# Causal convolution and two feed-forward layers in one fused kernel: the next tile's convolution moved to other slots, and another warm-up of TensorE

## The chip, the cores and the metric

One Trainium2 chip, one core. The metric is the device time of one launch in microseconds; the times are a median of runs. The other numbers come from one execution that was recorded by the profiler.

## The reference

A softmax-weighted causal filter of 7 taps per head runs over 4 sequences of 4096 positions of width 192 (8 heads of 24 channels). Its output goes through two layers, each with a wide hidden part of 2048; all is float32.

```
w = softmax(weight)                          # [8 heads, 7 taps]
a[b,s,h,:] = sum_k w[h,k] * x_pad[b,s+k,h,:] # 6 zeros ahead of each sequence
h = a.reshape(16384,192) @ w_in1             # 192 -> 2048
y = (h * cos(h)) @ w_out1                    # 2048 -> 192
h = y @ w_in2
out = (h * clip(h + 3, 0, 6) / 6) @ w_out2
```

## The kernel before

**Tiles, phases, slots.** The 16384 positions are cut into 32 tiles of 512. A tile has a phase of layer 1 (L1) and later a phase of layer 2 (L2). A phase has 8 slots (q = 0 to 7); a slot makes 2 of the 16 chunks of 128 hidden units. The order of phases is: tile 0 in L1, then for k = 1 to 31 a "turn" of L1 of tile k followed by L2 of tile k-1, then L2 of tile 31. Turns 2 to 30 are a hardware loop (`Fori`) on every engine. `Phase` tuples say what a phase does besides its own layer (`turn_phases`, line 292): `result` is the tile whose output it turns for the store, `convolved` the tile for which it makes the convolution.

**TensorE (PE).** Every operand is split into a high and a low part (the float32r type), and products of 64 rows, one in the lower and one in the upper half of the array, run side by side. A slot has 19 such pairs, 38 matmuls in all (`lower`, `upper`, lines 412 and 438): it makes the hidden chunks of slot q in `h_ps` and mixes the gated chunks of slot q-3 (`LAG`) into `acc` and `acc_tail`. `h_ps` has two buffers, so slot q starts with a wait for the gate of slot q-2 (line 419 and on, `g_ready`); slot 0 of a phase also waits for both low parts of its source (`source_waits`, `lo_ready`).

**ScalarE (ACT) and VectorE (DVE).** In L1 a slot is a chain of both: ACT copies `h_ps` to `pre` with rounding, DVE subtracts (`fraction`, L628), ACT takes the sine, DVE multiplies (`gated`, L639), ACT makes `g_hi`, GpSimd (POOL) makes `g_lo`. In L2 it is ACT (Relu), DVE (L642), ACT, POOL. Each engine works its queue in program order.

**The convolution of the next tile** is DVE's, between these. `load_x` on SyncE (SP) fetches 512 positions into `x_in` and `x_in_tail` by 6 DMAs; `turn_x(i)` waits for them (`x_loaded`) and transposes both (L657, L658) into `xT`; `put_halo` copies the 6 positions ahead (L672, L673); `conv_taps` has 14 steps, 7 taps for the 128 main and for the 64 tail channels, into `in_f` and `in_ftail` (L683, L687). Then ACT splits the high parts (`split_high`) and DVE the low ones (L695, L700). In the kernel before all of it stands in the L2 phase of a turn: transposes and halo in slot 0, three steps in each of the slots 1 to 4, two in slot 5, the split in slot 6 (`SPLIT_SLOT`), and `turn_result` (L664, L665) in slot 7 (`TURN_SLOT`).

**SP.** One queue of DMA issues, in program order. `load_x(i)` waits until tile i-1 has been transposed (`x_turned`); `store(i)` waits for the transposes of `turn_result(i)` (`o_turned`). In the loop, before:

```
with sp.Fori(2, TILES - 1) as k:
    load_x(k + 1)
    store(k - 2)
```

**Start.** The loads of the weights, the convolution of tile 0 on DVE, and on PE a warm-up of 10 products (`warm_up`, line 494) that starts once 9 of the 14 steps of tile 0 are done.

Of the kernel before, what the change touches and what calls it, by code (L numbers as in the profile page):

```python
# [14 lines left out]
P = 128  # L15
TOK = 512
LAG = 3
WARM_PRODUCTS = 10
WARM_STEP = 9
G_BUFS = 4  # L20
TWO_PI = float(np.float32(2 * np.pi))
HALF_PI = float(np.float32(np.pi / 2))
# [4 lines left out]

Phase = namedtuple("Phase", "layer tile base before number result convolved conv_from rate setup source")  # L30


def conv_moe_kernel(nc, x, weight, w_in1, w_out1, w_in2, w_out2, out):
# [17 lines left out]
    TILES = B * SEQ // TOK  # L51
# [42 lines left out]
    with ctx:  # L94
# [6 lines left out]
        def sem(name):  # L101
            return ctx.enter_context(nc.semaphore(name))
# [85 lines left out]
        w_exp = sem("w_exp")  # L188
        head_step = sem("head_step")
        taps_spread = sem("taps_spread")  # L190
        taps_ready = sem("taps_ready")
        const_ready = sem("const_ready")

# [55 lines left out]

        STEPS = [(t, part) for t in range(TAPS) for part in (0, 1)]  # L250
        DRAIN_SLOT = LAG
        SPLIT_SLOT = SLOTS - 2
        TURN_SLOT = SLOTS - 1
        TURNS = 19
        STEPS_AHEAD = 4
        L1, L2 = 0, 1
        SPLIT_EARLY = {"hi": 1, "twin": 2, "tail": 4, "low_main": 2, "low_tail": 5}
        SPLIT_AFTER_DRAIN = {"hi": 4, "twin": 4, "tail": 5, "low_main": 5, "low_tail": 6}
# [13 lines left out]
        def result_turn(ph):  # L272


            return ph.number if ph.before == L2 and ph.layer == L2 else ph.number - 1
# [5 lines left out]
        def splits_of(ph):  # L281
# [4 lines left out]
                return ph.tile  # L286
            return ph.tile + 1 + (ph.source == L2)

        def first_phase():
            return Phase(L1, 0, 0, None, 0, None, 1, 1, 2, 0, L2)  # L290

        def turn_phases(k):

            base = 2 * SLOTS * k - SLOTS
            first = isinstance(k, int) and k == 1
            last = isinstance(k, int) and k == TILES - 1
            return [Phase(L1, k, base, L1 if first else L2, 2 * k - 1, None, None, None, None,
                          1 if first else None, L1),
                    Phase(L2, k - 1, base + SLOTS, L1, 2 * k, None if first else k - 2,
                          None if last else k + 1, 1, 3, 2 if first else None, L2)]  # L300

        def last_phase():
            return Phase(L2, TILES - 1, END - SLOTS, L2, 2 * TILES - 1, TILES - 2, None, None, None, None, L1)

        def splits_last(ph, q):

# [4 lines left out]
        @block.sync  # L311
        def _(sp):
            def load_x(i):

                if not isinstance(i, int) or i > 0:
                    sp.wait_ge(x_turned, 2 * i)
                for b in range(BLOCKS_D):
                    sp.dma_start(chip_block(x_in, x_in_tail, b), dram_block(x_blocks, i, b)).then_inc(x_loaded, 16)

            def load_block(b):  # L320
                for dst, src in loads_of(b):
                    sp.dma_start(dst, src).then_inc(staged[buffer_of(b)], 16)

            def store(i):

                sp.wait_ge(o_turned, 2 * (i + 1))
                for b in range(BLOCKS_D):
                    sp.dma_start(dram_block(out_blocks, i, b),
                                 chip_block(o_blk, o_blk_tail, b)).then_inc(o_stored, 16)

            sp.dma_start(w_soft[:, :], weight).then_inc(w_loaded, 16)
            load_x(0)
            for b in range(6):
                load_block(b)
            load_x(1)
            for b in (6, 7):
                sp.wait_ge(wlo_done, b - 5)
                load_block(b)
            for b in (8, 9):
                sp.wait_ge(wlo_done, b - 1)  # L340
                load_block(b)
            load_x(2)
            for b in range(10, 2 * BLOCKS):
                sp.wait_ge(wlo_done, b - 1)
                load_block(b)
            with sp.Fori(2, TILES - 1) as k:
                load_x(k + 1)
                store(k - 2)
            for i in range(TILES - 3, TILES):
                store(i)  # L350
            sp.wait_ge(o_stored, 16 * (BLOCKS_D * TILES + 1))

        @block.tensor
        def _(pe):
# [121 lines left out]
            def phase(ph):  # L476
                for q in range(SLOTS):
                    left = mix_of(ph, q - 1) if q > 0 else None
                    if q == 0 and ph.setup != 0:
                        left = ph.before, 1 - pair_of(ph), SLOTS - LAG - 1  # L480
                    for i in range(TURNS):
                        lower(i, ph, q, ph.base + q, mix_of(ph, q))
                        upper(i, ph, q, ph.base + q, mix_of(ph, q), left)

            def last_mixes():
# [5 lines left out]
                for i in range(3):  # L491
                    upper(i, None, None, None, None, (layer, pair, SLOTS - 1))

            def warm_up():

                pe.wait_ge(whi_done, 1)
                pe.wait_ge(conv_step, WARM_STEP)
                for _ in range(WARM_PRODUCTS):
                    pe.matmul(h_ps[:, 1, TOK:W], win_hi[L1][:, 0:P], win_hi[L1][:, 0:TOK], start=True, stop=True)

            UP, LOW = slice(0, DT), slice(DT, P)
            spread_taps()
# [1 line left out]
            phase(first_phase())  # L504
            for ph in turn_phases(1):
                phase(ph)
            with pe.Fori(2, TILES - 1) as k:
                for ph in turn_phases(k):
                    phase(ph)
            for ph in turn_phases(TILES - 1):  # L510
                phase(ph)
            phase(last_phase())
            last_mixes()

# [1 line left out]
        def _(act):  # L516
# [54 lines left out]
            def phase(ph):  # L571
                for q in range(SLOTS):
                    slot = ph.base + q
                    if ph.setup == 0 and q < 2:
                        act.wait_ge(wlo_done, 3 + q)
                    before_gate(ph.layer, q, slot)
                    if ph.layer == L1:
                        cosine(q, SLOTS * ph.tile + q)
                    if ph.convolved is not None and q == SPLIT_SLOT:
                        act.wait_ge(conv_step, len(STEPS) * (ph.convolved + 1))  # L580
                        split_high(L1, L1)
                    if splits_last(ph, q):
                        act.wait_ge(acc_read, ph.number)
                        split_high(L2, L1)
                    high_part(q, slot, ph.setup != 0 or q >= G_BUFS)
                    if q == DRAIN_SLOT and ph.before is not None:
                        copy_low(ph.before, 1 - pair_of(ph), ph.base, ph.number)
                    if ph.layer == L1 and ph.setup != 0:
                        if q == hands_over(ph)["hi"]:
                            act.wait_ge(acc_read, 1 if ph.setup == 1 else ph.number - 1)  # L590
                            split_hi(L2, L2)
                        if q == hands_over(ph)["twin"]:
                            split_twin(L2, L2)
                        if q == hands_over(ph)["tail"]:
                            split_tail(L2, L2)
                    if ph.setup in SPLIT_IN and q in SPLIT_IN[ph.setup]:
                        weight_high(SPLIT_IN[ph.setup][q])
# [12 lines left out]
            phase(first_phase())  # L610
            for ph in turn_phases(1):
                phase(ph)
            with act.Fori(2, TILES - 1) as k:
                for ph in turn_phases(k):
                    phase(ph)
            for ph in turn_phases(TILES - 1):
                phase(ph)
            phase(last_phase())
            copy_low(L2, pair_of(last_phase()), END, 2 * TILES)

# [1 line left out]
        def _(dve):  # L622
# [80 lines left out]
            def phase(ph):  # L703
                for q in range(SLOTS):
# [7 lines left out]
                    else:  # L712
                        gated(L2, q, slot, None, True)
                    if ph.convolved is not None:
                        if ph.setup != 0 and q == 0:
                            turn_x(ph.convolved)
                            put_halo(ph.convolved)
                        n = (q - ph.conv_from) * ph.rate + (STEPS_AHEAD if ph.setup == 0 else 0)
                        if q >= ph.conv_from:
                            for m in range(n, min(n + ph.rate, len(STEPS))):  # L720
                                conv_taps(ph.convolved, m)
                        if q == SPLIT_SLOT:
                            split_low_main(L1, L1, ph.convolved - 1)
                            split_low_tail(L1, L1, ph.convolved - 1)
                    if q == DRAIN_SLOT and ph.before is not None:
# [10 lines left out]
                        split_low_tail(L2, L1, TILES - 1)  # L736
                    if ph.result is not None and q == TURN_SLOT:
                        turn_result(ph.result, result_turn(ph))

            dve.memset(half_pi[:, :], HALF_PI).then_inc(const_ready, 1)  # L740
            dve.memset(three[:, :], 3.0).then_inc(const_ready, 1)
# [27 lines left out]
            split_low_tail(L1, L2, 0)  # L769
            turn_x(1)  # L770
            put_halo(1)
            for n in range(STEPS_AHEAD):
                conv_taps(1, n)
            phase(first_phase())
            for ph in turn_phases(1):
                phase(ph)
            with dve.Fori(2, TILES - 1) as k:
                for ph in turn_phases(k):
                    phase(ph)
            for ph in turn_phases(TILES - 1):  # L780
                phase(ph)
            phase(last_phase())
            dve.wait_ge(o_turned, 2 * (TILES - 1))
            drain_acc(L2, pair_of(last_phase()), END, 2 * TILES)
# [66 lines left out]
```

## Time and profile before

| what | value |
|---|---|
| median of 3 runs | 2374.57 us (2373.44 to 2374.64) |
| the profiled execution | 2375.52 us, its span 2373.8 us |
| PE busy | 2286.3 us (96%), 19470 matmuls |
| DVE busy | 1851.5 us (78%) |
| ACT busy | 1705.8 us (72%) |
| POOL busy | 1468.8 us (62%) |
| DMA | 32.94 MB, mean 14 GB/s |

Busy times are shares of the span. PE overlaps its matmuls, so its busy time doesn't tell how dense they are; for that one counts them in a stretch. The chain of work that ended last gives PE 44% and DVE 19% of the span, and 22% to "issue", where nothing that the profile shows was waited for.

### The profile page before, as it was taken

What the parts mean: (1) busy time and instruction counts of PE and PEld (TensorE: products, weight loads), DVE (VectorE), ACT (ScalarE), POOL (GpSimd) and SP (SyncE); (2) the same over time, 40 slices, a digit from 0 to 9 for tenths busy, and PEclk for the clock granted to TensorE, in tenths of its full rate; (3) what the DMA queues carried; (4) which work ended last, traced back from release to release, by engine and by line L of the source; (5) the groups of instructions that cost most, each with busy time, mean ns of one, the idle gap of its engine ahead of it and who ended that gap; (6) DMA issues with size and microseconds to landing.
All of it is one profiled execution on the core that took longest, in us unless ns stands there. A gap on an engine that the chain in (4) does not pass through costs nothing.

```text
span 2373.8 us, 57021 instructions
## 1 busy us (share of the span) xinstructions
PE 2286.3 (96%) x19470; PEld 1997.7 (84%) x19470; DVE 1851.5 (78%) x2509; ACT 1705.8 (72%) x2836; POOL 1468.8 (62%) x1059
## 2 busy tenths in 40 slices
PE   5899999999999999999999999999999999999998
PEld 4789798888889888888898888998788988888886
DVE  8688877888877888777888778887778887788853
ACT  5876777766777667777667777677776677776674
POOL 6766666566566666566666665665666666656664
PEclk9999999999999999999999999999999999999999
DMA  4100000000000000000000000000000000000001
GB/s 109 37 8 15 0 13 13 13 13 7 7 13 13 13 13 0 13 13 13 13 9 4 13 13 13 13 0 13 13 13 13 12 1 13 13 13 13 2 7 21
DMA packets 208238, 32.94 MB, mean 14 GB/s; under 512 B 203088, under 2 KB 207184, under 8 KB 208208
## 3 DMA queue, kind: packets, MB, share of 16 engines
q1 hardware_dynamic: 208208, 32.53, 7.8%
q8 instruction: 20, 0.33, 0.1%
q14 instruction: 10, 0.08, 0.0%
HBM read 19.92 MB, written 12.58 MB: 14 GB/s over the span
## 4 chain that ended last, share of the span: by engine, by line
PE 44%; issue 22%; DVE 19%; POOL 9%; ACT 4%; DVEq 1%; POOLq 0%; SPq 0%; DMA 0%; ACTq 0%
PE h_ps L374 18%; PE acc L381 16%; PE acc_tail L388 11%; POOL g_lo L794 9%; DVE in_ftail L687 6%; DVE gate L642 5%; DVE in_f L687 4%; DVE in_f L683 1%; DVE in_tail L700 1%; ACT in_tail L558 1%; DVE in_ftail L651 1%; ACT in_hi L552 1%; ACT in_twin L555 1%; ACT pre L525 1%; ACT g_hi L540 0%
## 5 line engine op out<-in xcount | busy, mean ns | idle before, releaser
L794 POOL TENSOR_TENSOR g_lo<-gate,g_hi 128x512 fp32r<-128x512 f32 x1024 | 1428.9, 1417 | 857.1 <-ACT g_hi L540 855.7
L381 PE MATMUL acc<-g_hi,wout 64*128 64x512 f32 x4096 | 1429.9, 389 | 1.7 <-POOL g_lo L794 1.7
L374 PE MATMUL h_ps<-in_hi,win_hi 64*128 64x512 f32 x2048 | 808.3, 395 | 60.8 <-DVE in_tail L700 46.5
L540 ACT ACTIVATE g_hi<-gate 128x512 fp32r<-128x512 f32 x1024 | 613.7, 631 | 326.4 <-DVE gate L642 275.6
L381 PEld LDWEIGHTS acc<-g_hi,wout 64*128 64x128 f32 x4096 | 756.2, 185 | 66.4 <-issue 3.1
L388 PE MATMUL acc_tail<-g_lo,wout 64*128 64x512 f32 x2048 | 807.4, 394 | 0.0
L388 PE MATMUL acc_tail<-g_hi,wout 64*128 64x512 f32 x2048 | 805.6, 393 | 0.0
L374 PE MATMUL h_ps<-in_lo,win_hi 64*128 64x512 f32 x2048 | 803.2, 392 | 0.0
L374 PE MATMUL h_ps<-in_hi,win_lo 64*128 64x512 f32 x2048 | 800.3, 391 | 0.0
L381 PE MATMUL acc<-g_lo,wout 64*128 64x512 f32 x2048 | 800.2, 391 | 0.0
L374 PE MATMUL h_ps<-in_tail,wtail_hi 64*128 64x512 f32 x2048 | 798.1, 390 | 0.0
L628 DVE TENSOR_TENSOR pre<-pre,h_ps 128x512 f32<-128x512 int32 x512 | 334.6, 684 | 289.5 <-ACT pre L523 288.5
L374 PEld LDWEIGHTS h_ps<-in_hi,win_hi 64*128 64x128 f32 x2048 | 379.1, 185 | 109.8 <-issue 44.7
L525 ACT ACTIVATE pre<-h_ps,three 128x512 f32<-128x512 f32 x512 | 337.2, 683 | 163.8 <-PE h_ps L374 163.1
L642 DVE SCALAR_TENSOR_TENSOR gate<-pre,h_ps 128x512 f32<-128x512 f32 x512 | 332.6, 676 | 126.2 <-ACT pre L525 126.1
L388 PEld LDWEIGHTS acc_tail<-g_lo,wout 64*128 64x128 f32 x2048 | 376.5, 184 | 32.9
L374 PEld LDWEIGHTS h_ps<-in_hi,win_lo 64*128 64x128 f32 x2048 | 378.2, 185 | 27.6
L381 PEld LDWEIGHTS acc<-g_lo,wout 64*128 64x128 f32 x2048 | 376.3, 184 | 29.6
L374 PEld LDWEIGHTS h_ps<-in_lo,win_hi 64*128 64x128 f32 x2048 | 379.2, 185 | 24.8
L388 PEld LDWEIGHTS acc_tail<-g_hi,wout 64*128 64x128 f32 x2048 | 379.3, 185 | 24.5
L374 PEld LDWEIGHTS h_ps<-in_tail,wtail_hi 64*128 64x128 f32 x2048 | 378.6, 185 | 22.4
L533 ACT ACTIVATE pre<-pre,half_pi 128x512 f32<-128x512 f32 x512 | 349.1, 717 | 65.4 <-DVE pre L628 56.2
(72 smaller groups left out, 2359.3 us busy)
## 6 DMA issues: line engine op xcount, KB each, us to landing
x_in<-in_x SPq DMA_DIRECT2D x128, 64.0 KB, 2.2
out_dram<-o_blk SPq DMA_DIRECT2D x128, 64.0 KB, 1.8
blk_tail<-in_x SPq DMA_DIRECT2D x64, 64.0 KB, 2.2
out_dram<-blk_tail SPq DMA_DIRECT2D x64, 64.0 KB, 1.8
stage<-in_moe_w_out SPq DMA_DIRECT2D x6, 384.0 KB, 3.3
stage<-in_moe_w_in SPq DMA_DIRECT2D x3, 512.0 KB, 3.5
stage<-in_moe_w_in SPq DMA_DIRECT2D x6, 256.0 KB, 4.3
gate<-in_moe_w_out SPq DMA_DIRECT2D x2, 384.0 KB, 11.0
```

The costliest lines, as they stand in the source:

```text
L374: return pe.matmul(chunk_of(h_ps, q, half), w, x, start=start, stop=stop)
L381: return pe.matmul(acc[pair][:, :], wout[layer][rows, 2 * q + half, cols], g[rows, :], start=start, stop=stop)
L388: return pe.matmul(acc_tail[pair][:, :], wout[layer][rows, 2 * q + half, P:2 * P], g[rows, :], start=start, stop=stop)
L525: i = act.activation(p, h, ACT.Relu, bias=three[:, 0:1])
L533: act.activation(p, p, ACT.Sin, bias=half_pi[:, 0:1], scale=-TWO_PI).then_inc(cos_ready, 1)
L540: act.activation(chunk_of(g_hi, q, half), chunk_of(gate, q, half), ACT.Copy).then_inc(ghi_ready, 1)
L552: act.activation(in_hi[to][:, :], in_f[layer][:, :], ACT.Copy).then_inc(hi_ready[to], 1)
L555: act.activation(in_twin[to][DT:P, :], in_ftail[layer][:, :], ACT.Copy).then_inc(twin_ready[to], 1)
L628: dve.tensor_tensor(p, p.bitcast(I32), chunk_of(h_ps, q, half), ALU.subtract).then_inc(frac_ready, 1)
L642: dve.scalar_tensor_tensor(out=g, in0=p, scalar=6.0, in1=h, op0=ALU.min, op1=ALU.mult).then_inc(g_ready, 1)
L687: ins = dve.scalar_tensor_tensor(out=dst[:, :], in0=src[:, t:t + TOK], scalar=taps[0:rows, part, t:t + 1], in1=dst[:, :], op0=ALU.mult, op ...
L794: pool.tensor_tensor(chunk_of(g_lo, q, half), chunk_of(gate, q, half), chunk_of(g_hi, q, half).bitcast(F32), ALU.subtract).then_inc(glo_re ...
```

## The change

The transposes of a tile go to slot 7 of a phase (a new field `turned` of `Phase`): in the L2 phase of turn k it is tile k+2, right after `turn_result(k - 2)`. Its halo is put in slot 0 of the next L1 phase, its first four steps in the slots 1, 4, 6 and 7 of that phase, the other ten in the slots 0 to 4 of the L2 phase that follows (2, 2, 2, 1 and 3). `SPLIT_SLOT` is 5 instead of 6 (6 in the first phase). On SP the fourth load stands ahead of the loop, and in the loop the store comes first and then the load of tile k+2. The loops run to 29; turn 30 is written out. The warm-up waits for 7 steps instead of 9 and for two weight blocks instead of one, and issues 84 products of 64 rows, in pairs of lower and upper rows, instead of 10 of 128 rows.

```diff
-WARM_STEP = 9
+WARM_STEP = 7
+WARM_SERIES = 8
-Phase = namedtuple("Phase", "layer tile base before number result convolved conv_from rate setup source")
+Phase = namedtuple("Phase", "layer tile base before number result turned convolved setup source")
-        SPLIT_SLOT = SLOTS - 2
+        SPLIT_SLOT = SLOTS - 3
         TURN_SLOT = SLOTS - 1
+        CONV_FIRST = [4, 4, 6, 8, 10, 12, 14, 14, 14]
+        CONV = {0: [0, 0, 1, 1, 1, 2, 2, 3, 4], 1: [4, 6, 8, 10, 11, 14, 14, 14, 14]}
-        STEPS_AHEAD = 4
+        def conv_range(ph, q):
+            done = CONV_FIRST if ph.setup == 0 else CONV[ph.layer]
+            return range(done[q], done[q + 1])
+        def splits_convolved(ph, q):
+            return ph.convolved is not None and (ph.layer == L2 or ph.setup == 0) and q == split_slot(ph)
+        def split_slot(ph):
+            return SPLIT_SLOT + 1 if ph.setup == 0 else SPLIT_SLOT
         def first_phase():
-            return Phase(L1, 0, 0, None, 0, None, 1, 1, 2, 0, L2)
+            return Phase(L1, 0, 0, None, 0, None, 2, 1, 0, L2)
...
-            return [Phase(L1, k, base, L1 if first else L2, 2 * k - 1, None, None, None, None,
-                          1 if first else None, L1),
-                    Phase(L2, k - 1, base + SLOTS, L1, 2 * k, None if first else k - 2,
-                          None if last else k + 1, 1, 3, 2 if first else None, L2)]
+            more = None if last else k + 1
+            late = isinstance(k, int) and k + 2 >= TILES
+            return [Phase(L1, k, base, L1 if first else L2, 2 * k - 1, None, None, more, 1 if first else None, L1),
+                    Phase(L2, k - 1, base + SLOTS, L1, 2 * k, None if first else k - 2, None if late else k + 2,
+                          more, 2 if first else None, L2)]
...
@@ SyncE
-            with sp.Fori(2, TILES - 1) as k:
-                load_x(k + 1)
+            load_x(3)
+            with sp.Fori(2, TILES - 2) as k:
                 store(k - 2)
-            for i in range(TILES - 3, TILES):
+                load_x(k + 2)
+            for i in range(TILES - 4, TILES):
                 store(i)
@@ TensorE
+            def warm_unit(rows, moving):
+                dst = h_ps[:, 1, TOK:W] if rows is UP else acc[1][:, :]
+                return pe.matmul(dst, win_hi[L1][rows, HALF_FF - P:HALF_FF], moving[L1][rows, 0:TOK],
+                                 start=True, stop=True)
             def warm_up():
-                pe.wait_ge(whi_done, 1)
+                pe.wait_ge(whi_done, 2)
                 pe.wait_ge(conv_step, WARM_STEP)
-                for _ in range(WARM_PRODUCTS):
-                    pe.matmul(h_ps[:, 1, TOK:W], win_hi[L1][:, 0:P], win_hi[L1][:, 0:TOK], start=True, stop=True)
+                for _ in range(WARM_PRODUCTS + WARM_SERIES):
+                    for rows in (LOW, UP):
+                        warm_unit(rows, win_hi)
+                for _ in range(WARM_SERIES):
+                    warm_unit(LOW, win_hi)
+                    warm_unit(UP, wtail_hi)
+                for _ in range(WARM_SERIES):
+                    for rows in (LOW, UP):
+                        warm_unit(rows, win_hi).then_inc(warmed, 1)
+                for _ in range(WARM_SERIES):
+                    for rows in (LOW, UP):
+                        pe.wait_ge(whi_done, 2)
+                        warm_unit(rows, win_hi)
@@ ScalarE
-                    if ph.convolved is not None and q == SPLIT_SLOT:
+                    if splits_convolved(ph, q):
@@ VectorE
                     if ph.convolved is not None:
-                        if ph.setup != 0 and q == 0:
-                            turn_x(ph.convolved)
+                        if ph.layer == L1 and ph.setup != 0 and q == 0:
                             put_halo(ph.convolved)
-                        n = (q - ph.conv_from) * ph.rate + (STEPS_AHEAD if ph.setup == 0 else 0)
-                        if q >= ph.conv_from:
-                            for m in range(n, min(n + ph.rate, len(STEPS))):
-                                conv_taps(ph.convolved, m)
-                        if q == SPLIT_SLOT:
+                        for m in conv_range(ph, q):
+                            conv_taps(ph.convolved, m)
+                        if splits_convolved(ph, q):
                             split_low_main(L1, L1, ph.convolved - 1)
                             split_low_tail(L1, L1, ph.convolved - 1)
...
                     if ph.result is not None and q == TURN_SLOT:
                         turn_result(ph.result, result_turn(ph))
+                    if ph.turned is not None and q == TURN_SLOT:
+                        turn_x(ph.turned)
...
-            for n in range(STEPS_AHEAD):
+            for n in range(CONV_FIRST[0]):
                 conv_taps(1, n)
```

## Rows read from the trace of the kernel before

**Rows 1.** Waits of PE: engine line, what for; us in total, times, longest.

```profile
PE h_ps L374 <- DVE in_tail L700: 46.5, 33, 7.1
PE h_ps L374 <- DVE gate L642: 13.6, 30, 0.5
```

**Rows 2.** PE in order of time: start, duration, line, out<-in, [idle before <-releaser].

```profile
1019.21 0.48 PE L374 MATMUL h_ps<-in_hi,win_hi 64*128 64x512 f32 x1 [1.11 <-DVE in_tail L700]
...
1052.13 0.39 PE L374 MATMUL h_ps<-in_hi,win_hi 64*128 64x512 f32 x1
...
1056.52 0.39 PE L374 MATMUL h_ps<-in_hi,win_hi 64*128 64x512 f32 x1
...
1091.59 0.49 PE L374 MATMUL h_ps<-in_hi,win_hi 64*128 64x512 f32 x1 [1.13 <-DVE in_tail L700]
```

**Rows 3.** DVE and POOL in order of time, slots 2 and 3 of an L2 phase.

```profile
1069.31 0.73 DVE L687 SCALAR_TENSOR_TENSOR in_ftail<-xT_tail,taps,in_ftail 64x512 f32<-64x512 f32 x1
1069.98 1.78 DVE L687 SCALAR_TENSOR_TENSOR in_f<-xT,taps,in_f 128x512 f32<-128x512 f32 x1
...
1069.59 3.32 POOL L794 TENSOR_TENSOR g_lo<-gate,g_hi 128x512 fp32r<-128x512 f32 x2 [2.34 <-ACT g_hi L540]
```

**Rows 4.** Waits of SP's queue; then the page's DMA issues (KB each, us to landing).

```profile
SPq L328 <- DVE blk_tail L665: 2025.4, 32, 102.1
...
blk_tail<-in_x SPq DMA_DIRECT2D x64, 64.0 KB, 2.2
```

**Rows 5.** SP's DMA issues in order of time, around a loop end: start, duration.

```profile
1025.31 0.86 SPq L328 DMA_DIRECT2D out_dram<-blk_tail  x2
1026.98 1.94 SPq L318 DMA_DIRECT2D x_in<-in_x  x4
1029.10 0.88 SPq L318 DMA_DIRECT2D blk_tail<-in_x  x2
```

**Rows 6.** DVE in order of time: end of an L2 phase, then L1 slots 2 and 5.

```profile
1021.92 0.71 DVE L665 STREAM_TRANSPOSE blk_tail<-sum_tail 64x512 f32<-64x512 f32 x1
...
1032.58 1.28 DVE L628 TENSOR_TENSOR pre<-pre,h_ps 128x512 f32<-128x512 int32 x2 [1.71 <-ACT pre L523]
1034.07 1.30 DVE L639 TENSOR_TENSOR gate<-pre,h_ps 128x512 f32<-128x512 f32 x2 [0.20 <-ACT pre L533]
...
1046.65 1.28 DVE L628 TENSOR_TENSOR pre<-pre,h_ps 128x512 f32<-128x512 int32 x2 [1.70 <-ACT pre L523]
```

**Rows 7.** PE and DVE where the last phase, which has no convolution, ends.

```profile
2354.97 0.39 PE L388 MATMUL acc_tail<-g_lo,wout 64*128 64x512 f32 x1
...
2357.07 0.71 DVE L665 STREAM_TRANSPOSE blk_tail<-sum_tail 64x512 f32<-64x512 f32 x1
```

**Rows 8.** DVE in order of time: both transposes of a tile of x.

```profile
1060.16 0.70 DVE L657 STREAM_TRANSPOSE xT<-x_in 128x512 f32<-128x512 f32 x1
1060.79 0.66 DVE L658 STREAM_TRANSPOSE xT_tail<-blk_tail 64x512 f32<-64x512 f32 x1
```

**Rows 9.** Stretches: busy (count) of PE, PEld, DVE, ACT, POOL; PE clock; DMA.

```profile
68.77:72.50 3.73, 0.61 (x5) 0.18 (x1) 3.55 (x4) 3.68 (x8) 3.73 (x4) 0.84 0.36 105
72.50:78.10 5.60, 5.56 (x26) 4.45 (x28) 2.58 (x4) 3.90 (x6) 3.42 (x3) 0.50 0.00 0
...
110.20:113.50 3.30, 0.40 (x4) 0.00 (x0) 3.00 (x4) 2.96 (x6) 3.30 (x4) 1.00 0.00 0
```

**Rows 10.** PE, then DVE, in order of time: the start.

```profile
17.99 4.60 PE L499 MATMUL h_ps<-win_hi 128*128 128x512 f32 x10 [13.28 <-DVE in_f L687]
29.66 0.79 PE L374 MATMUL h_ps<-in_hi,win_hi 64*128 64x512 f32 x1 [7.07 <-DVE in_tail L700]
...
13.77 0.73 DVE L687 SCALAR_TENSOR_TENSOR in_f<-xT,taps,in_f 128x512 f32<-128x512 f32 x1
...
34.72 0.73 DVE L687 SCALAR_TENSOR_TENSOR in_ftail<-xT_tail,taps,in_ftail 64x512 f32<-64x512 f32 x1
...
37.09 0.69 DVE L628 TENSOR_TENSOR pre<-pre,h_ps 128x512 f32<-128x512 int32 x1 [1.03 <-ACT pre L523]
```

More of the change, by code:

```diff
@@ L190, in conv_moe_kernel @@
         taps_spread = sem("taps_spread")
+        warmed = sem("warmed")
         taps_ready = sem("taps_ready")
@@ L296, in turn_phases @@
             last = isinstance(k, int) and k == TILES - 1
-            return [Phase(L1, k, base, L1 if first else L2, 2 * k - 1, None, None, None, None,
-                          1 if first else None, L1),
-                    Phase(L2, k - 1, base + SLOTS, L1, 2 * k, None if first else k - 2,
-                          None if last else k + 1, 1, 3, 2 if first else None, L2)]
+            more = None if last else k + 1
[3 more added lines that the diff above has]
+                          more, 2 if first else None, L2)]
         def last_phase():
-            return Phase(L2, TILES - 1, END - SLOTS, L2, 2 * TILES - 1, TILES - 2, None, None, None, None, L1)
+            return Phase(L2, TILES - 1, END - SLOTS, L2, 2 * TILES - 1, TILES - 2, None, None, None, L1)
         def splits_last(ph, q):
@@ L506, in _ @@
                 phase(ph)
-            with pe.Fori(2, TILES - 1) as k:
+            with pe.Fori(2, TILES - 2) as k:
                 for ph in turn_phases(k):
                     phase(ph)
-            for ph in turn_phases(TILES - 1):
-                phase(ph)
+            for k in (TILES - 2, TILES - 1):
+                for ph in turn_phases(k):
+                    phase(ph)
             phase(last_phase())
@@ L612, in _ @@
                 phase(ph)
-            with act.Fori(2, TILES - 1) as k:
+            with act.Fori(2, TILES - 2) as k:
                 for ph in turn_phases(k):
                     phase(ph)
-            for ph in turn_phases(TILES - 1):
-                phase(ph)
+            for k in (TILES - 2, TILES - 1):
+                for ph in turn_phases(k):
+                    phase(ph)
             phase(last_phase())
@@ L776, in _ @@
                 phase(ph)
-            with dve.Fori(2, TILES - 1) as k:
+            with dve.Fori(2, TILES - 2) as k:
                 for ph in turn_phases(k):
                     phase(ph)
-            for ph in turn_phases(TILES - 1):
-                phase(ph)
+            for k in (TILES - 2, TILES - 1):
+                for ph in turn_phases(k):
+                    phase(ph)
             phase(last_phase())
```

## The prediction

> **What bounds the kernel now.** I read four views, in this order: the page, the waits of PE, PE in order of time over one turn, and then the queues of DVE and SP over the same turn. The waits name what PE stands for in the loop: the low part of the next tile's source, 33 times, and the gate of L2, 30 times [rows 1]. PE in order of time gives the price. A slot without a wait takes 1056.52 - 1052.13 = 4.39 us [rows 2], which is 0.116 us for each of its 38 matmuls. A turn of 16 such slots would be 70.3 us, and it is 1091.59 - 1019.21 = 72.4 us [rows 2]. So PE bounds the kernel, all but some 2.1 us of each turn, and those go to DVE: in the L2 phase a slot with three steps of the convolution is longer than PE's 4.39 us, since a step takes 0.73 us alone and 1.78 us where a `g_lo` of POOL runs already [rows 3]. DVE falls behind, the gate of slot 5 is 0.5 us late, and the split in slot 6 ends 1.1 us after PE wants it. 30 turns (k = 1 to 30) have this loss, about 62 us in all. That is the most that the moved steps can win in the loop.
>
> **Steps, halo and split.** Of the 14 steps an L2 slot now holds two at most in slots 0 to 2, one beside the drain, and three in slot 4. Two gates (2 x 0.6 us) and two steps, one alone and one behind POOL, make 1.2 + 0.7 + 1.7 = 3.6 us, under 4.39. Slot 4 has 1.2 + 0.7 + 2 x 1.7 = 5.3 us, so DVE ends it 0.9 us late; the gate may come almost two slots after its chunk before PE needs the buffer, and the split starts then, in slot 5, over one slot ahead of PE's demand. In L1 a slot has four DVE instructions of 0.65 us, 2.6 us of 4.39, and gets one thing more: the halo (four copies), a step, a low split, or the drain. A lone step starts before POOL's `g_lo` of that slot and takes 0.73 us, and POOL has the room to give it back. I price all this at nothing, and take the whole loss of 2.1 us off a turn. If the cover fails, it is by a step that starts behind POOL and costs 1 us more in L1; bounds for a turn: 2.1 us won, down to 1.0 us.
>
> **The transposes.** This is the part that I expect to decide. In the L2 phase of turn k, slot 7, DVE runs `turn_result(k - 2)` and then `turn_x(k + 2)`, which waits for the load of tile k+2. SP's program in turn k is `store(k - 2)` and then `load_x(k + 2)`, and the store waits for exactly that `turn_result`. SP does stand at that wait nearly all the time, 2025 us of the span [rows 4], so nothing lets the load go earlier. Before, the store stood there too, but the load behind it was needed only half a turn later. Now DVE waits, with its queue blocked, for six store issues, six load issues and a landing.
>
> Its length, from a turn of the kernel before, where the same issues follow each other: the result's transposes end at 1021.92 + 0.71 = 1022.63 [rows 6]; the last load issue ends at 1029.10 + 0.88 = 1029.98 and so starts at about 1029.6 [rows 5]; it lands 2.2 us later [rows 4], at 1031.8. That is 9.2 us. Between the store's last issue (ends 1026.17) and the load's first (1026.98) lies the loop's branch [rows 5], which is no longer there; of these 0.8 us I take 0.4 off. The wait is 8.8 us (bounds 8.3 and 9.3).
>
> Now against PE. Let T be the start of L1 slot 0. In the last phase, which has no convolution and therefore no lag, the slot after slot 7 starts at 2354.97 and the result's transposes end at 2357.78 [rows 7], at T + 2.8. The load has landed at T + 11.6, both transposes (1.3 us from 1060.16 to 1061.45 [rows 8]) end at T + 12.9. Only then can DVE take the first fraction of L1 slot 0, and from a first fraction to the end of a first gate it is 1034.07 + 0.69 - 1032.58 = 2.2 us [rows 6]: T + 15.1. PE needs that gate to start slot 2 at T + 8.8. With 0.1 us for the release, PE stands 6.4 us (bounds 5.7 and 7.1). ACT and POOL wait for the same fraction; nothing else on PE's queue can pass.
>
> **The clock.** After a stall of 3.7 us the granted clock fell, and the next 5.6 us of dense work were granted 0.50, the 1.2 GHz level: 26 matmuls instead of 5.6 / 0.116 = 48, so 5.6 - 26 x 0.116 = 2.6 us lost [rows 9]. A stall of 3.3 us left the clock at 1.00 [rows 9]. 6.4 us is longer than both, so I add 2.6 us a turn (bounds 0 and 3.5). It falls on slot 2 and a part of slot 3, where the chain of ACT and DVE has no lead to give.
>
> The Trainium skill, "TensorE: Matmul & The Clock Gate", section "Why this matters for your kernels", says the same of idle gaps between bursts of matmuls, and by it too each turn would pay anew; 110.2 to 113.5 us shows that a gap has to be long enough. The same notes, "DMA: Bandwidth & Descriptors", section "Rules for kernel authors", ask that a DMA be issued early and its semaphore be waited for late, so that the fixed cost overlaps. The trace before does that (DVE never waits for a load in the loop), and the change undoes it; that page's fixed cost of about 2 us for a DMA is close to the 2.2 us measured here from issue to landing, and an estimate with 2.0 would be 28 x 0.2 = 6 us lower.
>
> **How many turns.** The wait exists where a load stands behind a store: k = 2 to 29, 28 turns. In turn 1 tile 3 is loaded ahead of the loop, and in turns 30 and 31 nothing is transposed. Each of the 28 turns changes by + 6.4 + 2.6 - 2.1 = + 6.9 us, which is + 193; turns 1 and 30 win 2.1 each, - 4.
>
> **The start.** The warm-up now starts when step 7 is done, at 14.5 us instead of 18.0 [rows 10]. Its 42 pairs take 0.43 us each at 1.2 GHz and 0.23 us at 2.4 [rows 9, 2]: 9.7 us if all were fast, 18 us if all were slow; with 13 slow ones, as in the 5.6 us above, 12.3 us, to 26.8. PE's first real product waits for the split until 29.66 anyway [rows 10], so the warm-up is hidden unless it is slow throughout (then 2.9 us late). Before, the first phase began at the lower level. At the higher one its first chunk comes 2 us earlier, but DVE is at the steps of tile 1 until 35.45 and takes the first fraction then, as it does now; only the 1.03 us that it waited for the second chunk goes [rows 10]. Behind this the chain of ACT and DVE sets the pace of the first phase. I take - 1 us (bounds - 4 and + 3). The last step of tile 1 and its split stay where they were, so PE's stall at 68.8 us stays.
>
> **The sum.** The profiled execution took 2375.5 us (span 2373.8 and 1.7 around it): 2375.5 + 193 - 4 - 1 = 2563.5; the median is 0.9 lower, so 2563 us, + 8%.
>
> **Rivals.**
> A. *The clock stays up.* As the forecast without the 2.6 us a turn: 2563 - 73 = 2490. If the stall is broken up enough for that, the slots after it cost something too, since gates of slots 2 to 5 come 14.07 / 3 = 4.69 us apart in L1 [rows 6], 0.3 us over PE's slot, and after a stall the lead that covered this is gone: up to 2510. For it: the 3.3 us case; against it: 6.4 us is nearly double.
> B. *ACT and DVE don't catch up.* The same 0.3 us over some five slots binds in the forecast's case as well, 1.4 us a turn: 2563 + 39 = 2602. Against it: the slow clock already gives that chain 2 us of lead in slot 2.
> C. *The load is not late* (the other side). If the wait for tile k+2 were met when DVE reaches it, only the gain stays: 30 x 2.1 + 1 off 2374.6 is 2311. It decides as soon as the load's landing comes before T + 4.5 or so, that is if SP issued it before the store. For it: before, DVE never waits for x in the loop. Against it: the order in SP's program, and the store's own wait on `turn_result`.
> D. *Half of it.* The stall is as said, but the gain of the moved steps is only 1.0 us a turn, as POOL's `g_lo` holds steps in L1: 2563 + 31 = 2594.
>
> **Chances.** Forecast 0.62, A 0.11, B 0.09, D 0.11, C 0.05, others 0.02. The bounds of stall (0.7 us) and clock (0.9 us) are 20 and 25 us over 28 turns, so the forecast's own range is 2530 to 2595. The range takes in most of A, B and D, 2505 to 2605. What this kernel's measurement can tell is about 0.2%, 5 us. Faster is C and a rest: 0.06; same 0.01; slower 0.93.
>
> **What would show it.** DVE's first transpose L657 waits for the DMA into `blk_tail` some 28 times, 8 to 9 us each, some 245 us in all; PE waits for the gate L639 28 times, 6 us each; the wait for L700 at 46.5 us falls to about 15, that for L642 to nothing; the granted clock is 0.50 for some 5 us in each turn, the mean about 0.97; the period of a turn is 79.3 us. The step on the transposes is wrong if L657 doesn't wait, the one on the clock if it stays at 1.00 behind the stall, the one on the steps if waits for L642 or L700 remain in the loop, and the one on the start if PE's first product of L1 comes after 30 us.

## The result and the profile after

| | before | changed |
|---|---|---|
| median | 2374.01 us (4 runs) | 2546.99 us (4 runs, 2545.54 to 2548.56) |
| ratio | 1 | 1.073, 95% interval 1.071 to 1.075 |
| span of the profiled execution | 2373.8 us | 2544.6 us |
| mean granted clock of PE | 0.997 | 0.959 |

The forecast was 2563 us, with 2505 to 2605. The changed kernel is 7.3% slower.

The waits of the changed kernel (engine, line, what for: us in total, times, longest) answer to [rows 1]:

```profile
DVE xT L693 <- DMA blk_tail<-in_x: 252.0, 29, 9.4
PEld h_ps L392 <- DVE gate L675: 185.5, 32, 7.0
PE h_ps L392 <- DVE gate L675: 172.2, 31, 6.6
...
PE h_ps L392 <- DVE in_tail L736: 11.5, 3, 4.6
...
SPq L345 <- DVE blk_tail L701: 2219.4, 32, 122.1
```

L736 is L700 of the kernel before, the low split: PE waits for it three times, all before the loop, and the gate of L2 is gone from PE's waits. So the moved steps do what they are for. In their place PE waits some 6 us for L675, the gate of L1, and DVE waits some 9 us for a DMA, both once in a turn.

One turn shows how the two belong together. DVE, then SP, then PE of the changed kernel, in order of time (start, duration, line):

```profile
1009.32 0.71 DVE L701 STREAM_TRANSPOSE blk_tail<-sum_tail 64x512 f32<-64x512 f32 x1
1018.98 0.71 DVE L693 STREAM_TRANSPOSE xT<-x_in 128x512 f32<-128x512 f32 x1 [8.95 <-DMA blk_tail<-in_x]
1019.61 0.66 DVE L694 STREAM_TRANSPOSE xT_tail<-blk_tail 64x512 f32<-64x512 f32 x1
1020.20 1.24 DVE L664 TENSOR_TENSOR pre<-pre,h_ps 128x512 f32<-128x512 int32 x2
1021.63 1.30 DVE L675 TENSOR_TENSOR gate<-pre,h_ps 128x512 f32<-128x512 f32 x2 [0.19 <-ACT pre L568]
```

```profile
1010.47 1.99 SPq L345 DMA_DIRECT2D out_dram<-o_blk  x4
1012.64 0.91 SPq L345 DMA_DIRECT2D out_dram<-blk_tail  x2
1014.03 2.00 SPq L335 DMA_DIRECT2D x_in<-in_x  x4
1016.21 0.88 SPq L335 DMA_DIRECT2D blk_tail<-in_x  x2
```

```profile
1015.84 0.39 PE L399 MATMUL acc<-g_hi,wout 64*128 64x512 f32 x1
1022.38 0.79 PE L392 MATMUL h_ps<-in_hi,win_hi 64*128 64x512 f32 x1 [6.15 <-DVE gate L675]
```

The result's transposes end at 1010.03, and only 0.44 us later SP issues the first of six stores. The six loads follow, and 1.9 us after the last of them has been issued DVE goes on, 8.95 us late by the profile. The first gate of L1 then ends at 1022.3, and PE starts its slot 2 at once. It was due 0.23 us after the row at 1015.84, at 1016.07: a stall of 6.3 us.

Stretches of the same turn (busy time and count of PE, PEld, DVE, ACT, POOL, then PE's granted clock), to be held against [rows 9]:

```profile
1015.90:1022.30 6.40, 0.33 (x4) 0.00 (x0) 3.13 (x6) 1.34 (x2) 0.00 (x0) 0.79 0.28 45
1022.40:1026.40 4.00, 4.00 (x20) 3.10 (x22) 2.92 (x9) 3.52 (x7) 2.53 (x2) 0.50 0.00 0
1026.40:1085.30 58.90, 58.90 (x512) 55.94 (x510) 46.42 (x61) 45.49 (x75) 39.79 (x28) 1.00 0.00 0
```

The clock fell during the stall (mean 0.79) and was at the 1.2 GHz level for 4 us of work behind it: 20 matmuls instead of 4.0 / 0.116 = 35. Slot 2 takes 6.34 us for it (slot 3 starts at 1028.72) instead of 4.39. The last row before the stall starts at 1015.84 here and at 1094.39 in the next turn, so a turn takes 78.5 us; it took 72.4 [rows 2]. Over the 28 turns that have the stall the mean is 78.5 us as well, 6.3 of it the stall and 2.0 the slow work behind it.

### The profile page after: what moved, and what is told of

It is laid out like the page before. It is cut to its first block, busy times and chain, and to the rows that moved or that the text cites. A ratio compares the mean times of both kernels' runs of the same rounds, so it can differ in the third digit from the quotient of the medians.

```text
span 2544.6 us, 56934 instructions
## 1 busy us (share of the span) xinstructions
PE 2338.9 (92%) x19544; PEld 2029.5 (80%) x19544; DVE 1779.4 (70%) x2509; ACT 1724.3 (68%) x2836; POOL 1487.4 (58%) x1059
## 4 chain that ended last, share of the span: by engine, by line
PE 79%; SPq 6%; DVE 6%; issue 4%; ACT 3%; DMA 2%; DVEq 0%; ACTq 0%
PE h_ps L392 36%; PE acc L399 25%; PE acc_tail L406 18%; SPq L345 3%; SPq L335 3%; DMA blk_tail<-in_x 2%; ACT pre L568 1%; DVE gate L675 1%; DVE pre L664 1%; DVE o_blk L700 1%; DVE blk_tail L701 1%; ACT pre L560 1%; DVE in_ftail L723 0%; DVE in_f L723 0%; ACT g_hi L575 0%
## 5 line engine op out<-in xcount | busy, mean ns | idle before, releaser
L830 POOL TENSOR_TENSOR g_lo<-gate,g_hi 128x512 fp32r<-128x512 f32 x1024 | 1446.8, 1436 | 1011.0 <-ACT g_hi L575 1010.6
L399 PE MATMUL acc<-g_hi,wout 64*128 64x512 f32 x4096 | 1455.4, 395 | 1.7 <-POOL g_lo L830 1.7
L392 PE MATMUL h_ps<-in_hi,win_hi 64*128 64x512 f32 x2048 | 821.5, 402 | 183.7 <-DVE gate L675 172.2
L399 PEld LDWEIGHTS acc<-g_hi,wout 64*128 64x128 f32 x4096 | 772.2, 189 | 62.5 <-issue 3.5
L406 PE MATMUL acc_tail<-g_lo,wout 64*128 64x512 f32 x2048 | 819.1, 400 | 0.0
L392 PE MATMUL h_ps<-in_lo,win_hi 64*128 64x512 f32 x2048 | 815.9, 399 | 0.0
L399 PE MATMUL acc<-g_lo,wout 64*128 64x512 f32 x2048 | 814.0, 397 | 0.0
L392 PE MATMUL h_ps<-in_hi,win_lo 64*128 64x512 f32 x2048 | 812.8, 397 | 0.0
L392 PE MATMUL h_ps<-in_tail,wtail_hi 64*128 64x512 f32 x2048 | 810.2, 396 | 0.0
L560 ACT ACTIVATE pre<-h_ps,three 128x512 f32<-128x512 f32 x512 | 348.3, 686 | 289.3 <-PE h_ps L392 289.3
```

Of the source, the lines that this page charges most:

```text
L392: return pe.matmul(chunk_of(h_ps, q, half), w, x, start=start, stop=stop)
L399: return pe.matmul(acc[pair][:, :], wout[layer][rows, 2 * q + half, cols], g[rows, :], start=start, stop=stop)
L406: return pe.matmul(acc_tail[pair][:, :], wout[layer][rows, 2 * q + half, P:2 * P], g[rows, :], start=start, stop=stop)
L560: i = act.activation(p, h, ACT.Relu, bias=three[:, 0:1])
L830: pool.tensor_tensor(chunk_of(g_lo, q, half), chunk_of(gate, q, half), chunk_of(g_hi, q, half).bitcast(F32), ALU.subtract).then_inc(glo_re ...
```

## The experiments

Eight kernels were run. Their medians are to be read beside the kernel before on the same chip: 2375.6 us in e1 to e4, 2375.9 us in e5 to e8.

### The load ahead of the store

```diff
             with sp.Fori(2, TILES - 2) as k:
-                store(k - 2)
                 load_x(k + 2)
+                store(k - 2)
```

> The changed kernel with one swap in SyncE's loop: the load of tile k+2 is issued before the store of tile k-2. Theory (DVE waits for a load that stands behind the store): DVE's wait for the DMA in front of the transposes goes from 252 us to under 3, PE's waits for the gate L675 from 172 us to nearly 0, the clock is back near 0.99, and only the gain of the moved steps is left: 2374 - 30 x 2.1 = 2311 us, plus some 4 us for the longer stall in turn 1 (5.05 against 3.38 us, then a slow clock): 2315 us, 2305 to 2325. Rival (the steps in L1 or the transposes in slot 7 delay the chain of ACT and DVE by themselves): over 2400 us, with PE still waiting for L675 in each turn.

Measured: 2315.88 us (2311.97 to 2317.0), ratio to before 0.974 (0.9725 to 0.9758), clock 0.995. Its waits of PE and DVE:

```profile
PE h_ps L392 <- DVE in_tail L736: 12.0, 3, 4.6
...
PE h_ps L392 <- DVE gate L675: 0.7, 2, 0.4
...
DVE xT L693 <- DMA blk_tail<-in_x: 2.6, 1, 2.6
```

Two lines of SyncE's program are worth 231 us (233 if each kernel is taken against the kernel before that ran beside it). The wait for the DMA is left only at the very start, and that for L675 is 0.7 us in the whole run. With it the change is a gain of 2.6% over the kernel before: theory held, the rival (steps and transposes delay the chain by themselves) fell.

### The transposes two slots later, SyncE's order as changed

```diff
-                        if ph.layer == L1 and ph.setup != 0 and q == 0:
+                        if ph.layer == L1 and ph.setup != 0 and q == 1:
+                            turn_x(ph.convolved)
                             put_halo(ph.convolved)
...
-                    if ph.turned is not None and q == TURN_SLOT:
-                        turn_x(ph.turned)
...
-        CONV = {0: [0, 0, 1, 1, 1, 2, 2, 3, 4], ...
+        CONV = {0: [0, 0, 0, 1, 1, 2, 2, 3, 4], ...
```

> The changed kernel, SyncE's order as it is, but the transposes and the halo of the next tile stand in slot 1 of the L1 phase instead of slot 7 and slot 0, and its first step in slot 3. DVE reaches them about T + 11.6 us (T is PE's start of that phase), when the load has just landed (T + 11.6). Theory (only the place of the wait matters): DVE's wait for the DMA is under 1 us a turn, 2315 to 2335 us, a little over the swap since slot 1 now has 2.6 us of extra DVE work. Rival (the load is late by itself, or the steps in L1 cost the time): over 2400 us.

Measured: 2315.29 us (2314.75 to 2316.61). DVE's and PE's waits:

```profile
DVE xT L693 <- DMA blk_tail<-in_x: 5.3, 12, 2.5
...
PE h_ps L392 <- DVE gate L675: 0.4, 1, 0.4
```

(The first step stands in slot 2, not in slot 3 as the expectation has it.) The load is issued behind the store, just as in the changed kernel, and DVE meets it when it has landed: 5.3 us of waits in the whole run, 2.5 of them at the start. So neither the order of the two transfers nor the load's own length costs anything; the wait in front of a queue that had other work did. The 2.6 us more DVE work in slot 1 cost nothing against the swap (2315.9), which I had put a little higher.

### The stall filled with matmuls

```diff
+            def filler(ph):
+                pe.wait_ge(acc_read, ph.number - 1)
+                for _ in range(FILL_PAIRS):      # 26
+                    for rows, dst in ((LOW, acc), (UP, acc_tail)):
+                        pe.matmul(dst[pair_of(ph)][:, :], win_hi[L1][rows, 0:P], win_hi[L1][rows, 0:TOK],
+                                  start=True, stop=True)
...
                 for q in range(SLOTS):
+                    if q == 2 and ph.layer == L1 and ph.setup is None:
+                        filler(ph)
```

> The changed kernel; in L1 slot 2 of turns 2 to 29 PE issues 26 pairs of products of 64 rows on spare accumulators ahead of its wait, 26 x 0.23 = 6.0 us of work in a stall of 6.1 us, so PE isn't idle but is as late. Theory (stall 6.1 us and clock 2.1 us a turn are two terms): the clock is near 0.99, 2547 - 27 x 2.1 + 6 (turn 2, which has no stall to fill) = 2496 us, 2485 to 2510. Rival (the slow clock is hidden in the lag of ACT and DVE behind the stall, 0.3 us a slot): no gain or under 20 us, 2525 to 2555.

Measured: 2521.0 us (2518.5 to 2523.8), clock 0.996: 26 us less than the changed kernel for 26 pairs more in each turn. That lies between both expectations. The clock term is real, but only a part of it can be had back. The filler's condition holds in turn 31 too, where no tile has been awaited: the trace has its 52 products in 30 turns, 2 to 31, not in 2 to 29. PE of this kernel, the last of the fill and slot 2, then slot 6 of an L1 phase:

```profile
1013.32 0.39 PE L500 MATMUL acc_tail<-win_hi 64*128 64x512 f32 x1
1013.98 0.50 PE L393 MATMUL h_ps<-in_hi,win_hi 64*128 64x512 f32 x1 [0.27 <-DVE gate L686]
...
1031.44 0.39 PE L407 MATMUL acc_tail<-g_hi,wout 64*128 64x512 f32 x1
1032.01 0.50 PE L393 MATMUL h_ps<-in_hi,win_hi 64*128 64x512 f32 x1 [0.17 <-DVE gate L686]
```

The clock costs 78.5 - 70.3 - 6.3 = 1.9 us a turn in the changed kernel (2.0 by the means above). With it gone, a turn is 77.2 us (mean of the 28 turns, by the starts of slot 0), 1.3 us less. The other 0.6 or 0.7 us is in rows that wait. Slot 2 is as late as without the fill, 6.3 us in the mean, so the up to 0.4 us between the fill and the gate are no loss of their own. In slot 6 PE is held again, by 0.34 us here, since at full speed it has caught up with ACT and DVE, whose slots are longer than PE's there [rows 6]; the rest is 0.1 us or less in each of the slots around. So the rival of this run was a part of the truth, about a third of the term: what the slow clock takes, the chain would take otherwise.

The sum closes. 28 turns at 1.3 us are 37 us; turns 2 and 31 have no stall to fill and take 5.9 us longer each, by the starts of their slots; 37 - 12 = 25 us, and the two profiled executions differ by 25.1. Without what the fill costs in those two turns the clock would be worth 37 us.

### The warm-up alone

The kernel before with `warm_up` and `WARM_STEP` of the changed one, nothing else.

> The kernel before with the warm-up of the changed kernel alone. Theory (the warm-up ends 4 us before PE's first real product, and the clock falls again): within 1 us of before, 2373 us (2370 to 2375). Rival (the warm-up is worth what it is long for, a first phase at 2.4 GHz): 2369 or less, with no stretch at the lower level after 29.7 us.

Measured: 2375.31 us against 2375.62, ratio 0.9996 (0.9986 to 1.0005): no change. PE, then a stretch (columns as above):

```profile
25.78 0.39 PE L498 MATMUL h_ps<-win_hi 64*128 64x512 f32 x1
30.03 0.79 PE L376 MATMUL h_ps<-in_hi,win_hi 64*128 64x512 f32 x1 [3.86 <-DVE in_tail L718]
```

```profile
29.90:36.40 6.50, 6.37 (x22) 5.13 (x23) 6.33 (x12) 0.61 (x2) 3.83 (x4) 0.50 0.45 129
```

The last units of the series take 0.39 us, at full speed, and are over by 26.2 us. Then PE idles 3.86 us, and the first phase begins at 0.50 all the same.

### A warm-up that ends in time

Both have the load ahead of the store and the step of turn 1 moved (next experiment), and `WARM_STEP` 8 or 9 in place of 7: PE's extra products begin when that many steps of tile 0 are done.

> The kernel of e5_turn1 with WARM_STEP 8: the warm-up begins at 15.0 us instead of 13.3 and, 12.3 us long, ends at 27.3, so PE idles 2.4 us instead of 4.2 ahead of its first product. Theory (the idle time behind the warm-up is what drops the clock): the clock stays at the higher level through the first phase or most of it, and since DVE and ACT pace that phase, 0.5 to 1.5 us off e5_turn1. Rival (the first phase is paced by PE): 4 to 5 us off.

> As e7_warm8 with WARM_STEP 9: the warm-up begins at 16.7 and ends at 29.0, 0.7 us ahead of the first product. Theory: high clock through the first phase, PE's first product still at 29.7 us, 1 to 2 us off e5_turn1. Rival (a later end delays the first product): up to 1 us longer than e7_warm8.

Measured: 2313.78 and 2312.63 us (5 runs each), beside 2313.23 with step 7. With 8 the clock still falls, at 30.7 us; with 9 it holds through the first products, and the first of them comes no later (29.88 us, beside 30.10 with step 7). The same two stretches with step 7 and with step 9:

```profile
29.90:36.40 6.50, 6.30 (x21) 5.09 (x22) 6.38 (x12) 0.69 (x2) 3.89 (x4) 0.50 0.41 124
36.40:39.50 3.10, 3.10 (x20) 2.57 (x17) 1.86 (x3) 2.46 (x4) 0.00 (x0) 0.94 1.01 178
```

```profile
29.90:36.40 6.50, 6.50 (x36) 5.11 (x36) 6.43 (x12) 1.36 (x3) 3.71 (x4) 1.00 0.42 136
36.40:39.50 3.10, 1.78 (x9) 1.44 (x10) 1.69 (x3) 2.89 (x6) 1.01 (x1) 0.99 1.02 163
```

At 2.4 GHz PE does 36 matmuls instead of 21 by 36.4 us, and then it waits: DVE is busy for 6.4 of those 6.5 us in both. The higher clock with step 9 lasts only until 39.5 us. Behind PE's wait of 1.32 us for the first gate (it goes on at 37.80) the clock was at the lower level for 3.4 us:

```profile
39.50:43.00 3.50, 3.50 (x15) 3.01 (x14) 3.21 (x6) 3.02 (x6) 1.52 (x2) 0.52 0.11 18
```

The stall that ends the first phase still begins 1.3 us earlier (67.3 instead of 68.6 us), but these are not kept: the clock falls behind that stall, and slot 0 of turn 1 takes 7.22 us with step 9 and 4.49 with step 7. Behind the next stall it falls with step 7 and not with step 9. The profiled executions end 1.2 us apart, the medians 0.6, within their scatter, and where the clock happened to fall is as much a part of it as the warm-up. A faster PE gives next to nothing here, because DVE sets the pace of the first phase. The rivals (4 to 5 us, or a delay) fell. So did the expectation of step 8, that the clock stays up, and the 1 to 2 us that I expected of step 9.

### The step of turn 1

In the changed kernel the stall before L2 of tile 0 had grown from 3.4 to 5.05 us.

```diff
+        CONV_TURN1 = [0, 0, 1, 1, 1, 2, 2, 2, 4]
```

> The swapped kernel (load ahead of store); in turn 1 alone the step that stood in L1 slot 6, ahead of the low split of the source of L2, stands in slot 7. Theory (that one step waits behind a g_lo of POOL and delays the split by its 1.8 us): PE's stall at 109 us falls from 5.05 to about 3.4 us, the clock behind it stays low for 3.4 us or not at all; 1.7 to 3 us off the swapped kernel, 2313 us. Rival (the stall is the chain of ACT and DVE in turn 1, whatever the step): 5.0 us as before, 2316 us.

Measured: 2313.23 us (2312.79 to 2314.07), clock 0.997. The cause in the swapped kernel, DVE:

```profile
110.98 1.80 DVE L723 SCALAR_TENSOR_TENSOR in_f<-xT,taps,in_f 128x512 f32<-128x512 f32 x1
112.81 1.63 DVE L736 TENSOR_TENSOR in_tail<-in_ftail,in_tail 64x512 fp32r<-64x512 f32 x1
```

A convolution step, itself behind a `g_lo`, stands ahead of the split that PE waits for. PE around this stall, in the swapped kernel and with the step moved:

```profile
109.45 0.39 PE L406 MATMUL acc_tail<-g_hi,wout 64*128 64x512 f32 x1
114.50 0.79 PE L392 MATMUL h_ps<-in_hi,win_hi 64*128 64x512 f32 x1 [4.62 <-DVE in_tail L736]
...
108.44 0.39 PE L407 MATMUL acc_tail<-g_hi,wout 64*128 64x512 f32 x1
111.82 0.79 PE L393 MATMUL h_ps<-in_hi,win_hi 64*128 64x512 f32 x1 [2.96 <-DVE in_tail L737]
```

From start to start it is 5.05 us, and without the step 3.38, 1.7 less; the low clock around its end lasts 3.4 us instead of 6.8. The theory held for the stall. The median is 2.6 us less, but the single runs of the swapped kernel spread over 5 us, so this size is rough. Of the 3.8 us between the two profiled executions 1.5 are not the step's: in the swapped kernel the clock had also fallen at 72.6 us, behind the stall before, and slot 0 of L1 took 6.03 us instead of 4.49.

### Where the gain comes from

All 14 steps in the L2 phase, on top of the swap.

```diff
-        CONV = {0: [0, 0, 1, 1, 1, 2, 2, 3, 4], 1: [4, 6, 8, 10, 11, 14, 14, 14, 14]}
+        CONV = {0: [0] * 9, 1: [0, 3, 6, 9, 11, 14, 14, 14, 14]}
```

> The swapped kernel with all 14 steps in the L2 phase (3, 3, 3, 2, 3 in slots 0 to 4), the transposes in slot 7 and the halo in L1 slot 0 as in the changed kernel, the split in slot 5. Tells whether the gain of 2.0 us a turn is the earlier split or the four steps in L1. Theory (DVE's L2 slots with three steps are 1 us longer than PE's 4.39, and only a lead of 3.9 us covers it): the stall before L1 slot 0 (L736) stays away, the wait for the gate L678 comes back with 0.5 to 1 us a turn; 2316 + 30 x 0.7 = 2337 us, 2325 to 2350. Rival (the earlier split is all of the gain): no wait for L678, 2314 to 2319.

Measured: 2313.74 us (2312.99 to 2314.71). My expectation (2337) was wrong, the rival right: PE's wait for the gate of L2 is 0.2 us in all. DVE in this kernel, the gates of slots 1 to 5 of an L2 phase:

```profile
1037.87 1.27 DVE L678 SCALAR_TENSOR_TENSOR gate<-pre,h_ps 128x512 f32<-128x512 f32 x2
...
1043.14 1.27 DVE L678 SCALAR_TENSOR_TENSOR gate<-pre,h_ps 128x512 f32<-128x512 f32 x2
...
1048.40 1.27 DVE L678 SCALAR_TENSOR_TENSOR gate<-pre,h_ps 128x512 f32<-128x512 f32 x2
...
1053.16 1.26 DVE L678 SCALAR_TENSOR_TENSOR gate<-pre,h_ps 128x512 f32<-128x512 f32 x2
...
1058.42 1.27 DVE L678 SCALAR_TENSOR_TENSOR gate<-pre,h_ps 128x512 f32<-128x512 f32 x2
```

A slot with three steps takes DVE 5.27 us, 0.9 over PE's; slot 3, two steps and the drain, takes 4.76. From slot 1 to slot 5 the lag grows by 20.55 - 4 x 4.39 = 3.0 us, and PE's lead of almost two slots covers it. The kernel before had three steps and the drain in slot 3:

```profile
1073.38 1.27 DVE L642 SCALAR_TENSOR_TENSOR gate<-pre,h_ps 128x512 f32<-128x512 f32 x2
...
1079.84 1.27 DVE L642 SCALAR_TENSOR_TENSOR gate<-pre,h_ps 128x512 f32<-128x512 f32 x2
```

There one slot takes 6.46 us, 1.2 more than one with three steps alone, and DVE comes to the split a slot later. So the gain of 2 us a turn is had with the transposes and the halo out of L2's slot 0, which lets the steps begin a slot earlier, the split in slot 5, and two steps beside the drain, all three together. No run took them one at a time, so how much each is worth is not shown. The four steps in L1 bring nothing; one of them costs the 1.7 us of turn 1.

## Why the prediction was right, point by point

**The transposes.** Right, and it decided the sign. Forecast: DVE waits 8.8 us, goes on at T + 11.6, first gate at T + 15.1, stall 6.4 us. Measured with T = 1007.3 (slot 2 due at 1016.07, less two slots of 4.39): 8.95 us, T + 11.7, T + 15.0, 6.3 us. The 28 turns are the 29 waits for the DMA less the one at the start. PE stands in the turn after the one in which DVE runs into the wait, so its stalls are in turns 3 to 30.

**The clock.** Right in kind, mis-sized: 2.6 us a turn forecast, 2.0 measured. I had taken a case in which the clock fell 1.2 us before PE went on [rows 9] (a mean of 0.84 over 3.73 us); here it falls in the stall, some 2.8 us before (the level was 0.50 from 1019.6 to 1026.4), and 4 us of slow work are left instead of 5.6. In the 28 turns it stayed low for 6.8 us each time. 0.6 x 28 = 17 us are the larger part of what the forecast was too high.

**The steps and the split.** Right: 2.1 us a turn forecast, and with the wait removed 2375.6 - 2315.9 = 60 us, 62 forecast. A turn fell from 72.4 us to 70.3 in each turn of the loop. Rival C had this time, 2311 us, and the point from which it decides; its condition, the load ahead of the store, is what the first experiment made. I credited the gain to the whole spread of the steps; with all 14 steps in L2 nothing of it is lost, so it lies in the earlier start, the earlier split and the one step less beside the drain.

**Turn 1.** Missed: I had it 2.1 us faster, and it is 0.5 us slower (78.7 us from slot 0 to slot 0, 78.2 before). I did not look at what the moved steps stand in front of there. Its stall grew by 1.7 us, and the clock fell around its end.

**The start.** Forecast - 1 us, measured nothing. That step 7 would be done at 14.5 us was wrong (12.2 us in the changed kernel, where the long step of 2.8 us is the eighth and not the sixth). Nor did the series wait for the step: it began at 13.3, by the profile when ACT had split the second weight block, and ended 4 us too early. I had this gap at 2.9 us and still booked a fast first phase. The reason why it would not matter, DVE busy throughout, was right.

**The sum.** By the starts of slot 0 the 28 turns grew by 28 x (78.55 - 72.37) = 173 us, 193 forecast. Turn 2, which has no stall, wins 2.1, turn 1 loses 0.5, and start and end win 0.5: 171 us, and 2375.5 + 171 is the 2546.4 us of the profiled execution.

Rival A (the clock stays up) was tried by the filler: without the lower clock the kernel is 26 us faster, or 37 without the cost of filling turns 2 and 31, not 73. The clock term was only 2.0 us a turn, and the chain of ACT and DVE takes a part of that. Rival B's lag is there only when the clock is up. D has no trace: no wait came back in the loop.

## What to carry to other kernels

Before an instruction that waits for a transfer is moved, follow the issuing queue backwards from that transfer: if a wait stands ahead of it for something that the moved instruction's own engine does just before, the whole issue and landing time becomes a stall. A part that is idle for half a turn in the old schedule (SP at its store) says nothing about the new one.

A stall of the matrix engine is priced twice, by its length and by the slow work behind it, but the second price is read from where in the stall the clock falls, and partly hides a lag of other engines.

If a change loses, split it: here the moved steps won about 60 us and an issue order lost 231.

## What the runs showed that I had not expected

A step of the convolution took 0.73 us (0.48 for the first) where it started before POOL's `g_lo`, and 1.8 us where it started behind one; in L1 the steps mostly found the gap, and the halo's four copies took 0.17 us each in the changed kernel, against 1.1 us for the first of them before.

The granted clock held through a PE stall of 3.4 us at 110 us in the kernel before, and fell at the end of one of 3.4 us at 108.4 us in e5_turn1, where it was at 0.50 for 3.4 us from 111.9 us on. The same length of gap does not always have the same price. In e7_warm8 it even fell at 30.7 us, 0.7 us after PE had gone on from an idle time of 2.46 us, and in e8_warm9 at 39.5 us behind one of 1.32. The two stretches, e5_turn1 behind its stall:

```profile
111.90:115.30 3.40, 3.40 (x16) 2.75 (x18) 3.14 (x6) 2.51 (x5) 2.25 (x2) 0.51 0.00 0
```

and e7_warm8 behind its short gap:

```profile
30.70:37.50 6.80, 6.80 (x26) 5.46 (x27) 6.15 (x11) 1.80 (x3) 2.95 (x4) 0.50 0.63 157
```
